# Attention jobs placed two in a row between the large products, one result lying in a product's own bank

## What is computed

```python
def _attn_ref(q, k, v, beta):          # B=4, H=8, S=768, D=48
    k_n = k / (np.linalg.norm(k, axis=-1, keepdims=True) + 1e-06)
    state = np.zeros((B, H, D, D), dtype=np.float32)
    for t in range(S):
        kt, vt, bt = (k_n[:, :, t], v[:, :, t], beta[:, :, t, None])
        y[:, :, t] = np.einsum('bhd,bhde->bhe', q[:, :, t], state)
        v_old = np.einsum('bhde,bhd->bhe', state, kt)
        state = state + bt[:, :, :, None] * np.einsum('bhd,bhe->bhde', kt, vt - v_old)
    return y

def _moe_ref(x, w_in, w_out):          # 3072 tokens, 384 -> 2048 -> 384
    h = x @ w_in
    g = np.maximum(h, 0.0) + np.log1p(np.exp(-np.abs(h)))
    return g @ w_out
# _moe2_ref is the same with g = h * np.cos(h)
```

## Time and profile before

| | us |
|---|---|
| median of 3 runs | 1024.22 (1022.62 to 1024.91) |
| the profiled execution, its own time | 1021.11 |
| its span in the profile | 1019.1 |
| PE busy in the span | 970.8 (95%) |
| DVE busy | 728.9 (72%) |
| ACT busy | 515.9 (51%) |
| POOL busy | 333.5 (33%) |

### The profile page before, as it was taken

How to read it: one execution, slowest core, us unless ns; L and a number is a source line. 1 busy time by engine, 2 the same in 40 slices (tenths; PEclk the granted TensorE clock), 3 DMA queues, 4 the chain that set the end, 5 groups by cost and what they waited for, 6 DMA issues and landing times.

```text
span 1019.1 us, 24417 instructions
## 1 busy us (share of the span) xinstructions
PE 970.8 (95%) x10472; PEld 801.1 (79%) x10472; DVE 728.9 (72%) x1122; ACT 515.9 (51%) x848; POOL 333.5 (33%) x417
## 2 busy tenths in 40 slices
PE   4778899999999999999999999999999999999998
PEld 3676678778877778787788887888888888888897
DVE  4978775778587768755744676777868878688775
ACT  3564564563456355435644545545555455454543
POOL 2079458802950692088000596100100001001000
PEclk9769899999999999999999999999999999999999
DMA  9313123102110310011003421000101102010011
GB/s 206 65 33 96 32 49 64 48 5 43 37 48 17 57 39 17 18 34 48 13 5 95 158 90 62 1 1 9 54 1 30 34 2 61 1 26 7 1 32 31
DMA packets 110682, 42.55 MB, mean 42 GB/s; under 512 B 89040, under 2 KB 105936, under 8 KB 110576
## 3 DMA queue, kind: packets, MB, share of 16 engines
q1 hardware_dynamic: 105984, 39.73, 15.6%
q10 hardware_dynamic: 4592, 1.28, 0.6%
HBM read 31.56 MB, written 9.44 MB: 40 GB/s over the span
## 4 chain that ended last, share of the span: by engine, by line
PE 77%; DVE 11%; POOL 5%; ACT 4%; issue 2%; DMA 0%; SPq 0%; DVEq 0%; POOLq 0%
PE wide L1622 8%; PE wide L1624 7%; PE wide L1623 7%; PE wide L1646 6%; PE wide L1648 6%; PE wide L1647 6%; PE bank L1646 5%; PE bank L1648 4%; PE bank L1647 4%; PE bank L1624 4%; PE bank L1623 4%; PE bank L1622 4%; POOL inv L532 3%; POOL blk L529 2%; DVE g_lo L1199 2%
## 5 line engine op out<-in xcount | busy, mean ns | idle before, releaser
L1622 PE MATMUL wide<-x_hi,wi_hi 128*128 128x512 f32 x408 | 166.8, 409 | 0.9 <-DVE x_lo L983 0.9
L1199 DVE TENSOR_TENSOR g_lo<-tmp,g_hi 128x512 fp32r<-128x512 f32 x192 | 155.2, 808 | 6.6
L1623 PE MATMUL wide<-x_lo,wi_hi 128*128 128x512 f32 x408 | 159.8, 392 | 0.0
L1624 PE MATMUL wide<-x_hi,wi_lo 128*128 128x512 f32 x408 | 159.6, 391 | 0.0
L848 ACT ACTIVATE tmp<-wide 128x512 f32<-128x512 f32 x88 | 52.6, 598 | 196.2 <-PE wide L1624 195.9
L1190 DVE SCALAR_TENSOR_TENSOR tmp<-wide,tmp 128x512 f32<-128x512 f32 x88 | 60.6, 689 | 120.2 <-ACT tmp L852 119.9
L532 POOL TENSOR_TENSOR inv<-inv,blk 128x31 f32<-128x31 f32 (+15 forms) x155 | 119.4, 770 | 12.2
L1646 PE MATMUL wide<-g_hi,wo_hi 128*128 128x512 f32 x304 | 119.1, 392 | 0.0
L1648 PE MATMUL wide<-g_hi,wo_lo 128*128 128x512 f32 x304 | 119.0, 391 | 0.0
L1647 PE MATMUL wide<-g_lo,wo_hi 128*128 128x512 f32 x304 | 118.9, 391 | 0.0
L569 POOL TENSOR_TENSOR x_lo<-x_raw,x_hi 128x1536 fp32r<-128x1536 f32 x6 | 23.1, 3856 | 270.4 <-ACT x_hi L601 270.4
(11 more groups left out here) (181 smaller groups left out, 1869.4 us busy)
## 6 DMA issues: line engine op xcount, KB each, us to landing
stage<-in_moe_w_in SPq DMA_DIRECT2D x32, 192.0 KB, 3.1
stage<-in_moe_w_out SPq DMA_DIRECT2D x8, 768.0 KB, 4.9
qn<-in_q SPq DMA_DIRECT2D x24, 192.0 KB, 3.6
x_t<-x_res SPq DMA_DIRECT2D x6, 768.0 KB, 3.7
x_raw<-x_t SPq DMA_DIRECT2D x6, 768.0 KB, 4.9
res_v<-in_v SPq DMA_DIRECT2D x22, 192.0 KB, 3.7
out_x<-res SPq DMA_DIRECT2D x160, 24.0 KB, 1.5
kn<-in_k SPq DMA_DIRECT2D x32, 96.0 KB, 3.1
```

Source lines behind the costliest of these rows:

```text
L1199: nc.vector.tensor_tensor(lo, g, hi.bitcast(FP32), ALU.subtract).then_inc(g_ready, 1)
L1622: mm(dst, wi_hi[:, ft, kt, :], hi[:, kt, :], start=(kt == 0), stop=False)
L1623: mm(dst, wi_hi[:, ft, kt, :], lo[:, kt, :], start=False, stop=False)
L1624: last = mm(dst, wi_lo[:, ft, kt, :], hi[:, kt, :], start=False, stop=(kt == KT - 1))
```

## The change

The order of the jobs is rewritten so that at most places two jobs of PE follow one another directly, and the first job's first result gets a bank that it could not have before: one of the two banks of `product1`, that of step f, whose activation has been read by the time that place 2f comes. `LENT` names the jobs and places. Such a job waits on `h_used` of that step, and the `product1` that writes this bank next waits until the result has been fetched. Chunk 1 gets a generator of its own (`attention_1`). Computation, sizes and the number of matmuls stay.

After the change PE has (chunks 2 to 5): Q0 at 1, T1 at 5, P0 and M1 at 10, F1 and S1 at 12, T0 at 13, V0 and S0 at 14, SN0 at 16, KS1 and Y0 at 18, Q1 at 19, V1 and P1 at 20, SN1 at 22, YT0 at 23, KS0 of the next chunk and Y1 at 24, YT1 at 26. Chunk 1 has KS0 and P0 at 4 and M1 alone at 10. DVE has `take_inverse` at 6 and `turn_inverse` at 8 as before, the fetching of P0 and M1 at 10, of S1 at 12, of S0 at 15, of SN0 at 16, `take_blocks` at 17 (two parts) and 19 (two parts), the fetching of KS1 at 18. ACT has `take_outer` at 12 and, in tile 0, `high_weights(5)`, (6) and (7) at 14, 16 and 20. POOL's program is untouched.

```diff
+LENT_1 = {"KS0": 4, "M1": 10}
+LENT = {"P0": 10, "F1": 12, "V0": 14, "SN0": 16, "KS1": 18, "V1": 20, "SN1": 22}
+LENT_AHEAD = {"KS0": 24}
...
+def lend(c, job, at):
+    LENDER[CONTENT[c, job, 0]] = (c - 1) * FT + at // 2
...
+SLOTS = [n % 4 for n in range(BASE)]
+for _n in range(BASE, len(CONTENT)):
+    SLOTS.append(4 if _n in LENDER else sum(_m not in LENDER for _m in range(BASE, _n)) % 3)
...
+LOAN = {step: n for n, step in LENDER.items()}
...
     def await_room(eng, n):
-        if TURN[n]:
+        if n in LENDER:
+            eng.wait_ge(h_used, LENDER[n] + 1)
+        elif TURN[n]:
             eng.wait_ge(taken[slot(n)], TURN[n])
...
     def place(n):
-        return spare[slot(n)]
+        return bank[4 + ring(LENDER[n])] if n in LENDER else spare[slot(n)]
...
# ACT, chunk 1 (attention_1)
+            take_outer(1, 0)
+            take_outer(1, 1)
+            yield
+            take_transposes(2, "T0", knT[:, fill_of(2, 0)])
+            yield
+            high_weights(5)
+            yield
+            yield
+            act.wait_ge(inv_ready, 2)
+            high_weights(6)
+            yield
+            yield
+            take_y(1, "Y0")
+            yield
+            take_transposes(1, "Q1", qT)
+            yield
+            high_weights(7)
+            yield
...
# DVE, from place 15
             if after:
                 take_s(c + 1, 0, "S0")
             yield
             take_state(c, 0, "SN0")
             yield
             if after:
                 take_blocks(c + 1, 0)
                 take_blocks(c + 1, 1)
             yield
             take_rest(c, 1, "KS1")
             yield
             if after:
                 take_blocks(c + 1, 2)
                 take_blocks(c + 1, 3)
             yield
             take_delta(c, 1, "V1")
             yield
...
# PE, from place 10
+            scores(c, 0)
+            merge_inner(c, (0, 1))
+            yield
+            yield
+            merge_outer(c, (0, 1))
             if after:
                 gram(c + 1, 1)
             yield
...
@@ product1
             if before(n) is not None:
                 pe.wait_ge(h_used, before(n) + 1)
+            if n - 2 in LOAN:
+                await_taken(pe, LOAN[n - 2])
```

More of the change, by code:

```diff
@@ L224, in build @@
     filled, from_state = sem("filled"), sem("from_state")
-    taken = [sem(f"taken{i}") for i in range(4)]
+    taken = [sem(f"taken{i}") for i in range(4)] + [sem("lent_taken")]
     squared, norm_read, log_set, rooted, norm_step, kn_set = (
@@ L885, in _ @@
         for t in range(TILES - 1):
-            jobs = attention(t + 1)
+            jobs = attention(t + 1) if t else attention_1()
             for ft in range(FT):
@@ L1097, in first, with attention_1 @@
             low_weights(2)
+        def attention_1():
+            take_state(0, 1, "SN1")
+            yield
+            reduce(2)
+            yield
+            low_weights(3)
+            yield
+            factors(2)
+            yield
+            take_rest(1, 0, "KS0")
+            scale_keys(2)
+            yield
+            take_p(1, "P0")
+            yield
+            take_inverse(1)
+            yield
+            yield
+            turn_inverse(1)
+            yield
+            yield
+            take_inner(1, 0)
+            take_inner(1, 1)
+            yield
+            yield
+            take_s(2, 1, "S1")
+            yield
+            yield
+            take_delta(1, 0, "V0")
+            yield
+            take_s(2, 0, "S0")
+            yield
+            take_state(1, 0, "SN0")
+            yield
+            take_blocks(2, 0)
+            take_blocks(2, 1)
+            yield
+            take_rest(1, 1, "KS1")
+            yield
+            take_blocks(2, 2)
+            take_blocks(2, 3)
+            yield
+            take_delta(1, 1, "V1")
+            yield
+            take_p(1, "P1")
+            yield
+            take_state(1, 1, "SN1")
+            yield
+            take_x(1, 0, "YT0")
+            yield
+            take_rest(2, 0, "KS0")
+            yield
+            yield
+            take_x(1, 1, "YT1")
+            yield
+            yield
+            yield
+            yield
+            reduce(3)
+            yield
+            yield
         def attention(c):
             after = c + 1 < NCH
-            if c == 1:
-                take_state(0, 1, "SN1")
             yield
-            if c == 1:
-                reduce(2)
-            elif after:
+            if after:
                 factors(c + 1)
             yield
-            if c == 1:
-                low_weights(3)
             yield
-            if c == 1:
-                take_p(1, "P0")
             yield
-            if c == 1:
-                factors(2)
-            else:
-                take_p(c, "P0")
             yield
-            if c == 1:
-                scale_keys(2)
-                take_rest(1, 0, "KS0")
             yield
@@ L1529, in first, with attention_1 @@
             gram(1, 1)
+        def attention_1():
+            first_state()
+            yield
+            pe.wait_ge(q_loaded, 96)
+            transposes(1, "Q0", qn)
+            yield
+            gram(1, 0)
+            yield
+            yield
+            keys_on_state(1, 0, "KS0")
+            scores(1, 0)
+            yield
+            keys_transposed(2, 1)
+            yield
+            yield
+            yield
+            yield
+            yield
+            merge_inner(1, (0, 1))
+            yield
+            yield
+            merge_outer(1, (0, 1))
+            gram(2, 1)
+            yield
+            keys_transposed(2, 0)
+            yield
+            solve_values(1, 0, "V0")
+            gram(2, 0)
+            yield
+            yield
+            add_to_state(1, 0, "SN0")
+            yield
+            yield
+            keys_on_state(1, 1, "KS1")
+            read_out(1, 0, "Y0")
+            yield
+            pe.wait_ge(q_loaded, 128)
+            transposes(1, "Q1", qn)
+            yield
+            solve_values(1, 1, "V1")
+            scores(1, 1)
+            yield
+            yield
+            add_to_state(1, 1, "SN1")
+            yield
+            turn_out(1, "YT0", "Y0")
+            yield
+            keys_on_state(2, 0, "KS0")
+            read_out(1, 1, "Y1")
+            yield
+            yield
+            turn_out(1, "YT1", "Y1")
+            yield
+            yield
+            yield
+            yield
+            yield
+            yield
         def attention(c):
             after = c + 1 < NCH
-            if c == 1:
-                first_state()
             yield
```

143 lines of the change are left out of this document (81 added, 62 removed).

## The result

| | before | after |
|---|---|---|
| median of the runs, us | 1024.57 (1022.62 to 1025.78) | 1039.78 (1039.31 to 1040.58) |
| ratio of after to before | | 1.0151, 95% interval 1.0134 to 1.0169 |
| profiled execution, us (span) | 1021.11 (1019.1) | 1040.58 (1038.6) |
| mark to mark, tiles 0 to 3, us | 94.59, 93.28, 94.26, 89.42 | 105.28, 96.06, 95.80, 91.30 |
| mark to next gate, us | 66.8, 65.5, 66.4, 64.5 | 73.7, 67.4, 67.1, 65.8 |

A forecast was written before the change was run, and what follows sets the result against it. PE's own work was taken to bound the kernel, but late weights and blocks would make POOL hold each gate. Tile differences of 18.8 us plus 0.6 gave +19.4 on 1021.1, then 3.1 for the median: 1044, range 1039 to 1048.

The forecast's parts named there:

- The sum: Whole kernel: changes of the marks (first product of step 10) plus the end give +19.4 us, 1040.5; plus 3.1, 1044.
- POOL's start: POOL's scaling of the blocks begins 11.8 us behind the mark (first product of step 10), 19.9 in tile 0.
- Start + 49.5 + 5.3: Gate (second product of step 4) opens at POOL's start plus inversion plus take-over and activation: 66.6 us, tile 1 74.7.
- The natural arrival at 63.0: PE would reach the gate, step 4's second product, 63.0 us behind the mark if POOL let it; before, 65.5.
- over 20 us in total: Sign in the changed profile: PE's L1646 waits for the activation over 20 us, each followed by some 3 us slow clock.
- The pairs' 10 us: 27 pairs of small jobs in a row on PE save 0.38 us each, 10 us if nothing waits.
- (c): Rival: POOL's result isn't what the gate waits for and the pairs bring their 10 us: 1016, chance 0.06.
- Behind the gate: From gate to next mark: 27.8 us before, 28.2 after without the clock, including 1.0 for waits at F1 and T0.
- The clock: Half clock behind PE's wait at each gate costs 1.6 us, tile 0's as before and four new; bounds 0 and 2.
- (a): Rival: the same waits without half clock behind the four new gates, four times 1.6 us less: 1037.5, chance 0.2.
- (b): Rival: only chunk 2 is late, POOL makes up 3.5 us in the other tiles: about 1034, chance 0.07.
- (d): Rival: the pair doesn't save, its second job waits for banks or starts late; with longer waits 1052, chance 0.07.

The follow-up runs named there:

- The one part alone on the old order: Kernel before with only the high half of weight piece 7 made at ScalarE's place 20, not 17: ratio 1.0086.
- both parts undone: Changed kernel with the high weight halves at their old places and VectorE preparing the blocks early again, pairs kept: ratio 1.0053.
- undoing the blocks: Changed kernel with VectorE preparing the blocks directly behind the fetching of S0 and SN0, ahead of KS1's, weights still late: ratio 1.0143.
- three more edits: On the changed kernel with weights and blocks back: YT1's fetching behind step 14's activation (1.0027), read-outs one place later (1.0030), keys' scaling moved back (0.9997).
- the later versions: Cumulative edits on the changed kernel with weights and blocks back, such as read-outs one place later (1.0030), keys' scaling split off (0.9997), KS0 at place 28 (0.9984).
- the five versions with the same PE program: Changed kernel with weights back (1.0072), blocks back (1.0143), both (1.0053), both plus YT1's fetching later (1.0027), or most of POOL's inversion left out (0.9864).
- the version with the read-outs apart: Changed kernel with weights and blocks back and YT1's fetching later, plus read-outs Y0 and Y1 one place behind KS1 and KS0: ratio 1.0030.
- the three runs on its order: Kernel before with weight piece 7 late (1.0086), with blocks prepared late (1.0119), or with most of POOL's inversion left out (0.9886).
- the kernel before with late weights: Kernel before with only the high half of weight piece 7 moved from ScalarE's place 17 to 20: ratio 1.0086.
- the kernel before with late blocks: Kernel before with only VectorE's block parts moved from places 16 and 18 to 17 and 19: ratio 1.0119.
- the version with the factors in two parts: Version with weights and blocks back, YT1's fetching later and read-outs apart, plus scaling of the next keys behind step 2's activation: ratio 0.9997.

## Why the prediction was right, step by step

**The sum** was 19.4 us on one execution's own time, and between the two profiled executions it was 19.5. Between the medians it was 15.2. What failed is the last term, the 3.1 us added because the median of before lay that far above its profiled execution: the median of after lies 0.8 below its own. That puts the median at 1039.78 where 1044 was forecast, just inside the range. The kernel before was profiled in an execution 1.5 us faster than the fastest of its four runs, the changed one in the slowest of its four; the agreement to 0.1 us is luck in part. Marks came at 146.28, 251.56, 347.62, 443.42 and 534.72 for 145.4, 249.9, 346.3, 442.7 and 535.2. Its parts were 0.6, 9.9, 3.1, 2.1, 3.1 and 0.6, measured 1.5, 10.7, 2.8, 1.5, 1.9 and 1.1. The total is closer than its terms: errors cancelled.

**POOL's start**, the step that decided the sign, was right: 11.8 behind the mark forecast, 12.2 and 11.9 measured; 19.9 in tile 0, 19.6 measured. The one part alone on the old order gave 20.1. "Start + 49.5 + 5.3" gave 66.6 and 74.7, measured 67.4, 67.1 and 73.7. The causes were tried: with both parts undone the ratio falls from 1.0151 to 1.0053. But the number isn't the mechanism in every tile. In tile 3 DVE waited 0.92 us for POOL and PE not at all at the gate: its waits ahead of it in that stretch (1.14, 1.09, 0.69, 1.23) on top of 63.0 are 67.1 already.

**The natural arrival at 63.0** was right as PE's work and wrong as a time. With both parts undone the gate came at 66.0, and the four waits ahead of it in that stretch (0.38, 1.53, 0.18, 0.91) are 3.0. I had looked for what a late buffer would do at the gate, and not at the steps that the jobs were taken from. So the forecast "idle 3.6 us at the gate" was 0.99 in tile 2 and nothing in tile 3, and DVE's idle time was 1.82 and 0.92 and not some 3, and 5.15 in tile 1 and not near 12: the waits had been taken already, ahead of it. The sign "over 20 us in total" for L1811 came true with 22.9 us for another reason: the gates of tiles 1 to 4 hold 6.8 of it. In tile 1 I had said 12 us; PE waited 4.07 at the gate, and 63.0 + 1.46 (read-out) + 1.7 (half clock behind that) + 3.4 (three bare steps) + 4.07 is 73.6. That is also why the two parts undone bring less than they seemed to cost.

**The pairs' 10 us** was the term that was most over-sized. Six pairs took 1.1 to 1.3 us of PE's work from a stretch and not 2.3: some 0.2 each, half of the 0.38. The second job starts 0.97 us behind the first where V0 or V1 leads, 1.05 in KS1 and Y0, and 1.09 in P0 and M1 and in F1 and S1, and not 0.94 as the halves of a read-out do. V1 and P1 save 0.36. P0 and M1, each behind a bare place, had cost 1.19 and 1.18 and cost 2.27 as a pair: 0.10, or 0.2 with the longer product behind each job. This hardly showed in the total, since no gain of a pair ahead of the gate stood in the sum; it shows in rival (c).

**Behind the gate** 28.2 was forecast without the clock, and 28.64 and 28.66 measured in tiles 2 and 3. The forecast has a slip in it: its terms (+1.9, -1.3, -0.4, -0.4, +1.0) add up to +0.8 and not +0.4, which would have been 28.6 and 1.6 us more in the sum. F1's wait is 0.47 as forecast; T0's is 0.12, so the two cost 0.6 and not 1.0, and the smaller saving of the pairs made that up.

**The clock** was wrong in its places. Of four new stretches at half clock only one came, in tile 1, twice as long as I took it (6.6 us at 0.53), and one behind a wait that I had not foreseen. Together 4.5 us of work, against 6.4. The rule of the Trainium skill that the prediction quotes, page "TensorE: Matmul & The Clock Gate", section "HAM oscillation — how this bites in real kernels", held for the waits of 5.14 and 4.07 us and not for those of 0.99 and 1.76 at the gates of tiles 2 and 4. My sum had charged it at every gate, in tile 3 too, where PE didn't stop; the page ties it to the length of the gap, and I hadn't.

**The rivals.** (a) had the clock right in tiles 2 to 4 and not in tile 1. (b), that only chunk 2 is late, was wrong: undoing the blocks shortened each later stretch. (c), faster if POOL is in time, was worth its low chance and more doubt still: with POOL in time the kernel was 0.5% slower, and three more edits were needed to be even. (d) was half right: a pair saves half of what I took. Its longer waits for banks didn't come: F1's 0.47 is one for a lent bank, and the later versions add 0.6 at KS1 in tile 0 and 0.4, at most 0.7, at Q1 for the spare bank of KS1's second result.

## What to carry to other kernels

A small job between two large products isn't only a cost: it is the time in which the engine behind the products does its other work. Before packing such jobs together, add up for each step left bare what stands on the activation's engine ahead of the activation, and compare it with the two products' time. And when jobs move on one engine, look at what moves with them on the others: here an unrelated weight copy, three places later, cost 9 of the 15 us.

## What the runs showed of the hardware

**PE stops inside long rows of small matmuls.** With KS and a read-out in a row (192 small matmuls) PE waited 0.4 to 1.7 us inside the read-out, with no engine or transfer ending the wait, in the changed kernel and in the five versions with the same PE program at the same matmuls: 11, 35 and 8 before the end of Y1 of chunk 1, Y0 of chunk 2 and Y0 of chunk 3. In three of these versions Y0 of chunk 1 has one more, 0.9 to 1.3 us. PE's waits in the version with the read-outs apart have no such line; these are its first three:

```profile
PE bank L1811 <- DVE g_lo L1308: 12.0, 10, 4.9
PE bank L1355 <- DVE pT L982: 2.4, 1, 2.4
PE wide L1433 <- DVE tmp L1299: 1.8, 4, 0.5
```

A row of 192 isn't needed, though. The kernel before has the same kind of wait in the second matmul of the large product behind Y0 of chunk 3, where only a read-out's 128 stand in a row, and so have two of the three runs on its order (1.12 and 0.62 us):

```profile
338.73 0.39 PE L1647 MATMUL bank<-g_lo,wo_hi 128*128 128x512 f32 x1 [0.86 <-issue]
```

The places have something in common. Count PE's records in the trace (matmuls, weight loads and those of its sequencer) in order of their start, from 0. The waits in the read-outs of the changed kernel and its versions come at number 5314, 6337, 8130 and 10945, and the one of the kernel before at 10945 too. Each is 193 or 194 more than a multiple of 256. In the version with the read-outs apart, numbers 6337, 8129 and 10945 fall into read-outs as well, and PE doesn't wait. So both matter, a fixed point every 256 instructions and the row of small matmuls around it. That the supply of instructions is what runs out is the likeliest cause, not tried. The Trainium skill, page "Runtime: NRT & Kernel Launch", section "Instruction fetch mechanics", says that instructions are refilled in blocks of 256 and that crossing a block's end is mostly hidden. The trace agrees with both: in the changed kernel 49 of the 52 such points from 90 to 560 us show no wait. Where small matmuls of 15 ns each stand in a long row, some do.

**The clock doesn't follow the length of one wait.** Half clock stood behind waits of 1.46 us (174.08) and 4.07, and in the version with read-outs apart behind two of 0.62 and 0.92 close together; none stood behind 2.07 us at the gate of tile 1 of the kernel before with late weights (220.14), behind 1.91 at the last gate of the kernel before with late blocks, nor behind 1.14 at 354.10 and 0.99 at 318.98 of after, nor behind 0.62 and 0.96 close together in the version with the factors in two parts. Behind 3.85 us (165.97, late weights) it stood again. A wait of 1 to 2 us may or may not cost another 1.7; what decides between them stays open. The clock falls while PE still waits: ahead of the gate at 116.24 of after it was at 0.50 from 114 to 116 us.

**POOL slows DVE beside it.** With POOL at rest DVE's cast of 128x512 took 0.43 us and the subtraction behind it 0.69, 30 times each from 146 to 535 us of the kernel before. While POOL worked the cast took up to 1.93 and the subtraction up to 1.38. The longest casts stand beside POOL's scaling:

```profile
339.45 2.39 POOL L519 TENSOR_TENSOR blk<-blk,beta_blk 128x1024 f32<-128x1024 f32 x1 [23.00 <-DVE blk L941]
```
```profile
340.20 1.93 DVE L1197 CAST g_hi<-tmp 128x512 fp32r<-128x512 f32 x1
```

In the changed kernel PE's waits for the activation away from the gates came to 10.9 us, and with most of POOL's passes left out to 3.6 with the gates.
